# Rolling the middle groups of a two-layer expert kernel into a hardware loop

## The reference

```python
X = np.fft.fft(np.fft.fft(x, axis=1), axis=2).real          # 8 x 3072 x 256
# layer 1: cosine gate, temperature tau;  layer 2: linear gate w_gate
expert_idx = np.argmax(logits, axis=1)
gate_w = softmax(logits)[row, expert_idx]
for e in range(8):                                           # w1: 256 x 1024, w2: 1024 x 256
    h = np.maximum(x[mask] @ w1[e], 0.0)
    out[mask] = gate_w[mask, None] * (h @ w2[e])
```

## Time and profile before

| | |
|---|---|
| median of 3 runs | 2902.71 us (2898.22 to 2903.21) |
| the profiled execution | time 2902.71 us, span 2900.7 us |
| mean granted TensorE clock | 0.959 |
| TensorE matmul busy | 2682.5 us (92%), 22938 instructions |
| VectorE, ScalarE, GpSimd busy | 1317.6 us, 1168.6 us, 628.6 us |
| instructions in the span, sequencers' included | 64470 |

### The profile page before, as it was taken

The page is one execution under the profiler, slowest core; times in us unless marked ns, Lnnn a source line. Parts: engine busy times, 40 slices in busy tenths (PEclk is TensorE's granted clock), DMA queues, the critical chain, the costliest instruction groups (busy, mean ns, idle before and its releaser), DMA issues. The chain is left out here.

```text
span 2900.7 us, 64470 instructions
## 1 busy us (share of the span) xinstructions
PE 2682.5 (92%) x22938; PEld 2432.5 (84%) x22938; DVE 1317.6 (45%) x3980; ACT 1168.6 (40%) x2543; POOL 628.6 (22%) x639
## 2 busy tenths in 40 slices
PE   6777776499999999999999979999999999999998
PEld 5676675499899999999999968999999999999997
DVE  8888876144444444444444433333232323333332
ACT  3554455144443444444444423333343333333332
POOL 2445554211111111111111111111111111111111
PEclk9887897799999999999999989999999999999999
DMA  9567773426454536363545232254241523254220
GB/s 287 161 166 202 203 208 123 138 88 212 128 188 159 179 114 224 100 202 90 201 137 188 70 123 70 67 199 137 94 174 43 202 66 116 67 199 155 81 97 28
DMA packets 250174, 412.26 MB, mean 142 GB/s; under 512 B 41354, under 2 KB 192671, under 8 KB 236704
## 3 DMA queue, kind: packets, MB, share of 16 engines
q1 hardware_dynamic: 221568, 332.60, 36.8%
q0 software_dynamic: 28320, 75.94, 7.6%
HBM read 776.27 MB, written 133.29 MB: 314 GB/s over the span
## 5 line engine op out<-in xcount | busy, mean ns | idle before, releaser
L1139 DVE SCALAR_TENSOR_TENSOR m_hT_low<-m_hbank,m_hT_high 128x512 bf16<-128x512 f32 (+1 forms) x824 | 554.0, 673 | 1387.0 <-ACT m_hT_high L1252 1387.0
L1321 PE MATMUL m_hbank<-m_xT_low,up_high 128*128 128x256 bf16 (+1 forms) x3296 | 755.8, 272 | 0.0
L1323 PE MATMUL m_hbank<-m_xT_top,up_low 128*128 128x256 bf16 (+1 forms) x3296 | 746.0, 270 | 0.0
L1341 PE MATMUL m_ybank<-down_high,m_hT_low 128*128 128x264 bf16 (+1 forms) x3184 | 732.7, 278 | 0.0
L1343 PE MATMUL m_ybank<-down_low,m_hT_high 128*128 128x264 bf16 (+1 forms) x3184 | 728.8, 272 | 0.0
L1252 ACT ACTIVATE m_hT_high<-m_hbank 128x512 fp32r<-128x512 f32 (+1 forms) x824 | 480.2, 583 | 575.9 <-PE m_hbank L1323 575.7
L1318 PE MATMUL m_hbank<-m_xT_high,up_high 128*128 128x256 f32 (+1 forms) x3296 | 588.8, 301 | 6.0 <-DVE m_xT_low L1127 6.0
L1284 ACT ACTIVATE m_yr<-m_ybank,m_meta 128x264 f32<-128x264 f32 (+1 forms) x398 | 169.0, 474 | 778.7 <-PE m_ybank L1343 778.7
L1318 PEld LDWEIGHTS m_hbank<-m_xT_high,up_high 128*128 128x128 f32 x3296 | 443.2, 190 | 17.6 <-DVE m_xT_low L1127 7.2
L1338 PE MATMUL m_ybank<-down_high,m_hT_high 128*128 128x264 f32 (+1 forms) x3184 | 432.5, 288 | 1.0 <-issue 1.0
L1112 POOL DMA_INDIRECT records<-m_yr,m_idx x199 | 193.5, 972 | 1003.3 <-DVE m_idx L1197 915.6
(11 more groups left out here) (194 smaller groups left out, 2202.1 us busy)
## 6 DMA issues: line engine op xcount, KB each, us to landing
up_high<-w_high SPq DMA_DIRECT2D x210, 1024.0 KB, 6.4
down_high<-w_high SPq DMA_DIRECT2D x103, 1056.0 KB
up_low<-w_low SPq DMA_DIRECT2D x210, 512.0 KB, 8.3
down_high<-w_high SPq DMA_DIRECT2D x104, 1024.0 KB, 5.6
down_low<-w_low SPq DMA_DIRECT2D x103, 528.0 KB
down_low<-w_low SPq DMA_DIRECT2D x104, 512.0 KB, 7.0
m_xt<-records SPq DMA_DIRECT2D x192, 258.0 KB, 3.1
m_raw<-in_weights SPq DMA_DIRECT2D x66, 249.0 KB, 3.0
```

Source lines behind the costliest of these rows:

```text
L1139: nc.vector.scalar_tensor_tensor(hT_low[:, j % 2, 2 * i:2 * i + 2, 0:w], hbank[i][:].rearrange("p (c t) -> p c t", c=2)[:, :, 0:w], 0.0, h ...
L1321: nc.tensor.matmul(h, top_half(up_high[:, j % 2, at:at + P]), xT_low[:, c, 0:w], start=False, stop=False, skip_group_check=True)
L1323: done = nc.tensor.matmul(h, up_low[:, j % 2, at:at + P], xT_top[:, c, 0:w], start=False, stop=(c == 1), skip_group_check=True)
L1341: nc.tensor.matmul(y, hT_low[:, j % 2, c, rows], top_half(down_high[:, j % 2, cols]), start=False, stop=False, skip_group_check=True)
```

## The change

`groups` writes out the first and the last group and makes one hardware loop of the five between them, on each of the five engines and in both layers. The body inside the loop is the same 16 tiles; g is a register there. So each number waited for in it, each address into the tile table and each address of a weight piece is computed by the sequencer as it goes, and at the end of the body the sequencer branches back, 4 times in a layer and on each engine. Three conditions that ask for g == 0 are guarded because g is no longer always an integer.

```diff
                 def groups(eng, body):
-                    for g in range(NG):
-                        body(g, g == 0, g == NG - 1)
+                    body(0, True, False)
+                    with eng.Fori(1, NG - 1) as g:
+                        body(g, False, False)
+                    body(NG - 1, False, True)
...
-                        if not (g == 0 and j < 4):
+                        if not (isinstance(g, int) and g == 0 and j < 4):
                             dve.wait_ge(y_scaled, g * GROUP + (j - 3))
...
-                        if not (g == 0 and j == 0):
+                        if not (isinstance(g, int) and g == 0 and j == 0):
                             pe.wait_ge(xT_ready, g * GROUP + j)
...
-                            if not (g == 0 and j == 0):
+                            if not (isinstance(g, int) and g == 0 and j == 0):
                                 pe.wait_ge(hT_ready, g * (4 * GROUP) + (j * 4 + i - 3))
...
-                        if not (g == 0 and j == 0):
+                        if not (isinstance(g, int) and g == 0 and j == 0):
                             pe.wait_ge(y_scaled, g * GROUP + j)
```

## The result

| | before | after |
|---|---|---|
| median | 2902.32 us (4 runs, 2898.22 to 2903.21) | 2928.13 us (4 runs, 2925.6 to 2928.78) |
| profiled execution: time, span | 2902.71, 2900.7 us | 2932.91, 2930.9 us |
| mean granted TensorE clock | 0.959 | 0.955 |
| instructions in the span | 64470 | 69456 |

The loop makes the kernel 0.9% slower: ratio 1.009, 95% interval 1.0073 to 1.0107, or 25.8 us between the medians. The profiled execution of the new kernel is one of the longer ones, 30.2 us over that of before. Lines behind L1014 stand 2 further down than before (in the kernels of the experiments 3 to 8). The forecast was 2920 us, +17.6 us.

The account below looks back on a forecast made before the run. TensorE's work, fed by its own sequencer, was taken to bound both layers; 8 branches, each idling the array S - 0.79 = 2.2 us at S = 3.0, add 17.6 us to 2902.7, giving 2920 us, range 2902 to 2952.

Parts of the forecast that it names:

- the clock: TensorE behind branch stops: clock falls from 3.5 us idle on, adding 8 x 2.6 = 21 us; not in the 17.6 us.
- TensorE is the bound, and only its own sequencer matters: Both expert layers last as long as TensorE's work; other engines' losses cost nothing until they make TensorE idle.
- The cover of 2 us: TensorE's sequencer reads ahead of the array, so a stop costs only what exceeds some 2.0 us.
- Register work costs 0: Computed waits and addresses on every engine in the loops: cost 0, upper bound 1.3 us x 160 = 208 us.
- Each branch fetches its target: At 8 TensorE branches, a 13.0-packet group does not stay resident, so the sequencer stops for S to fetch; q8 packets unchanged.
- S = 3.0 us, idle S - 0.79: At each TensorE branch, fetch stop S is 3.0 us, a row load's median; idle 2.2 us, 8 times 17.6 us.
- the 0.50 for a resident target: The branch itself at the group's end, as seen in stage A without a fetch: 0.5 us in all.
- Other engines at their branches: Stops of VectorE, ScalarE, SyncE and GpSimd stay hidden, VectorE with 4.1 us of cover; cost 0 at S = 3.
- Covered: Rival at TensorE's branches: target held or prefetched, S under 1.5 us, not slower, 2903 to 2908 us; chance 0.25.
- Drained read-ahead: Rival in all 160 tiles: TensorE short by half of 1.3 us each, 104 us, 3007 us; chance 0.05.
- Long stop and slow clock: Rival at TensorE's branches: S from 4.3 to 7.5 us plus clock falls, 2952 to 2977 us; chance 0.13.
- the likeliest case: One stop at each TensorE branch, S between 1.5 and 4.3 us, no clock fall, 2909 to 2932 us; chance 0.53.

Follow-up runs that it names:

- the experiments 3 to 8: Follow-up kernels known only by number; the text given does not say which kernels bear these numbers.
- the pauses: Kernel before, no loops, TensorE's sequencer held at the same 8 places by 15, 26 or 35 semaphore increments; ratios 1.0021, 1.0089 and 1.0148.
- all_fetched_ahead_and_placed: Changed kernel plus prefetch hint on TensorE's, VectorE's and SyncE's branches, TensorE's loops placed with the branch mid-packet; 2934.44 us against 2934.55 before, ratio 0.9994.
- loop_on_tensor_alone: Changed kernel with the hardware loop on TensorE alone, the other four engines unrolled; 2922.34 us against 2897.19 before, ratio 1.0084.
- pauses_35: Kernel before, no loops, TensorE's sequencer held at the same 8 places by 35 increments of an unused semaphore; +43.4 us, ratio 1.0148.
- loops_without_tensor: Changed kernel with hardware loops on VectorE, ScalarE, GpSimd and SyncE, TensorE unrolled as before; 2899.15 us, ratio 1.0006 to the kernel before.
- the short loops: Kernel before, but TensorE loops tiles 4 to 11 of six full groups as two turns of 4 tiles, 12 branches; 2892.15 us against 2892.37, ratio 0.9999.
- the loops of one turn: Changed kernel with the five middle groups written out, each a loop of one turn, all engines, no branch back; 2897.26 us, ratio 1.0001 to before.

## Why the prediction was right, and where not

The forecast of 2920 us came with a range of 2902 to 2952, and 2928 lies in it. The mechanism was right; the idle time came out by two errors that cancel, and what lifts 2920 to 2928 is a term that the sum had at 0, the clock.

**TensorE is the bound, and only its own sequencer matters.** Right: looping the other four changed 0.06%, looping TensorE alone gave the whole loss.

**The cover of 2 us.** Right. It was read from one block of 3.07 us and one interval; the pauses, from 2.3 to 5.4 us, give 2.0.

**Register work costs 0.** Right: all_fetched_ahead_and_placed has all of it in place and ran at 0.9994 (0.9982 to 1.0006). TensorE's part was smaller than counted, 892 sequencer steps more in the span of the change (1951 against 1059), 5.6 a tile and not 12. SyncE's wait for ybank, 3.8 us a tile before, is still 3.7 (row of the new kernel):
```profile
SPq L1075 <- PE m_ybank L1345: 723.8, 198, 9.4
```

**Each branch fetches its target.** Right: 13 packets don't stay, 3.3 do, and with the hint and the placing the stop is gone (0.34 to 0.37 us). But q8 moved 187 packets and not as many as before (169): the fetches of the targets come on top. How many steps an engine keeps no run shows; the steps in the trace from branch to branch only bound it: TensorE stopped with 3463 and 3293 and didn't with 884; SyncE stopped with 718 and 597; VectorE stopped with 672 in layer 1 and not with 233 in layer 2 (next step after 0.3 us); ScalarE's 289 and 235 and GpSimd's 112 and 96 ran through.

**S = 3.0 us, idle S - 0.79.** Two errors that nearly cancel, so the forecast idle of 17.6 us against 17.0 measured is in part luck. Taken from the load of a tile's rows, S came out low: from ALU_OP to the first wait behind it the branches of layer 1 took 3.6 to 3.8 us and those of layer 2 4.1 to 4.6, and less the 0.50 for a resident target that is an S of 3.1 to 4.1, 3.5 in the mean. By the formula the idle would then be 2.7 us at a branch, and it was 2.12 (17.0/8). For from the first wait to the matmul it took 0.3 us and not 0.66, and from ALU_OP to the matmul all but 2.2 us was idle (at the first branch 919.77 to 923.79, 4.02 us, of which 1.77 idle), where the cover was put at 1.95. The load of rows was also the wrong likeness: the stop is a packet of about 1.3 us, with 1.0 us ahead of it and 1.4 us behind.

**The clock.** This is the term that was mis-sized. The prediction let the clock fall only from an idle spell of 3.5 us on, read from two gaps in stage A, and so gave it 0 in the sum. In the layers it fell behind 1.84 us once and behind all of 2.2 to 2.8 us in layer 2, 9.3 us in the profiled execution; in loop_on_tensor_alone it didn't fall behind 1.94 and 2.14 us of layer 1, and in pauses_35 not behind 3.32 and 3.42 us. Two gaps set no threshold. These 9.3 us and 2.1 us for the restarts come on top of the 17.0 and make 28.4 of the profiled execution's 30.2; the timed runs, at +25.8, had mean clocks of 0.956 to 0.958 instead of 0.955.

**Other engines at their branches.** Right for the sum. ScalarE didn't stop at all. VectorE's cover was put at 4.1 us, and the one stop of 5.7 us in loops_without_tensor came through with 1.48. In the changed kernel its longest stop was 5.0 us, and no row of TensorE's waits shows it: TensorE itself stood for 1.7 us there.

**The rivals.** "Covered" asked for S under 1.5 us, and no branch was that short (at 1.5 it costs 8 x 0.71 = 5.7 us, not 5.8). "Drained read-ahead" falls with all_fetched_ahead_and_placed and with the short loops. "Long stop and slow clock" had the clock fall, which came without the long stop. The time, 2928, lies in the likeliest case's own range of 2909 to 2932.

## What to carry to other kernels

Before rolling a loop, count a turn's steps on the engine that is the bound, here TensorE: turns of 884 steps were free, turns of 3293 and 3463 paid a stop of 3.3 to 4.3 us at each branch, less 2 us of read-ahead; no run lies between. The stops of the other engines reached TensorE only through VectorE, once in each of three runs, with 1.3 to 1.5 us. Where the body must be long, a prefetch hint on the branches of TensorE, VectorE and SyncE and TensorE's loop placed so that its branch is far from a packet's start gave the unrolled time back (ratio 0.9994). Price an idle spell of a busy TensorE at more than its length: the kernels with 16 us of idle and more lost 1.4 to 1.6 times their idle time (25.8 us for 17.0, 25.2 for 17.4, 23.5 for 17.1, 26.6 for 16.2, 43.4 for 27.1), those with less between 1.1 (9.4 for 8.2) and 2.1 times (5.8 for 2.7). And count the instructions of a control kernel in its profile before reading its time: the loops of one turn looked in the source as if they held the register work, and did not.

## What the runs showed of the hardware

- A taken branch of TensorE took 3.3 to 4.3 us where its target had to be fetched, 0.34 to 0.46 us with the hint, 0.21 to 0.24 us to code still there (short_loops_on_tensor, stage A); not taken 0.08 us. With the hint and a packet begun within 0.3 us of it, it took 2.0 to 2.5 us.
- A branch that had to fetch ended 1.3 to 1.5 us after its packet on the instruction queue had landed; the packet began 0.9 to 1.5 us into the branch and took 0.9 to 1.9 us (28 branches).
- Without the hint the next step of SyncE came 5.1 to 6.2 us behind its branch, that of VectorE in layer 1 2.8 to 5.7 us; with it 0.5 and 0.5 to 0.6 us. The branch record itself stays under 0.1 us there; on TensorE it holds the stop.
- The granted clock fell to half for 3.4 or 6.8 us behind 27 of the 40 idle spells of 1.8 us and more that a branch, a fetch or a pause made in an otherwise full stretch (19 of 21 in layer 2, 8 of 19 in layer 1), and behind none of the 18 shorter ones. A fall cost 1.6 us, the long one 2.9. Which spells it takes stays open: 1.84 us had a fall, 3.32 and 3.42 us had none.
- An increment of a semaphore took TensorE's sequencer 0.15 us (pauses_35), a wait that was already met 0.11 us (the kernel before), from one start to the next.
